# First batch of the FFT stages: A and the first tile's B moved from SBUF to SBUF instead of through memory

## What is computed

```python
# x: (4, 3008, 256); filt_r, filt_i: (1505, 256)
X = np.fft.rfft(x, axis=1)
y = np.fft.irfft(X * (filt_r + 1j * filt_i)[None], n=3008, axis=1)
x = y.reshape(12032, 256)
x = np.maximum(x @ w_in, 0.0) ** 2 @ w_out            # d_ff 2048
g = x @ w_gate                                        # d_ff 1536
out = (g / (1 + np.exp(-g)) * (x @ w_val)) @ w_out2
```

## Time and profile before

| | |
|---|---|
| median of 3 runs | 2358.94 us (2358.81 to 2359.14) |
| the profiled execution | 2358.64 us; span of its trace 2356.8 us |
| mean granted TensorE clock | 0.997 of full speed |
| TensorE (PE) busy | 2329.5 us, 99% of the span |
| weight loads (PEld) | 1903.6 us, 81% |
| VectorE, ScalarE, GpSimd busy | 68%, 54%, 3% |
| DMA | 153.74 MB, mean 65 GB/s |

### The profile page before, as it was taken

The page is one execution under the profiler, slowest core; times in us unless marked ns, Lnnn a source line. Parts: engine busy times, 40 slices in busy tenths (PEclk is TensorE's granted clock), DMA queues, the critical chain, the costliest instruction groups (busy, mean ns, idle before and its releaser), DMA issues.

```text
span 2356.8 us, 31292 instructions
## 1 busy us (share of the span) xinstructions
PE 2329.5 (99%) x10581; PEld 1903.6 (81%) x10581; DVE 1601.1 (68%) x2707; ACT 1272.7 (54%) x2468; POOL 61.2 (3%) x124
## 2 busy tenths in 40 slices
PE   8899999999999999999999999999999999999999
PEld 4688888888888888888888878888888888888887
DVE  3567766677666776566555777777777777777776
ACT  4566656566655665555544445555555555555554
POOL 0100000000000000000000000000000000000000
PEclk9899999999999999999999999999999999999999
DMA  9643433333333333101002101001011011010000
GB/s 270 207 132 96 129 96 107 91 107 112 101 98 99 99 106 122 29 27 42 27 19 72 50 1 36 23 14 36 1 36 36 1 36 36 1 36 28 10 19 18
DMA packets 95423, 153.74 MB, mean 65 GB/s; under 512 B 10080, under 2 KB 48416, under 8 KB 94976
## 3 DMA queue, kind: packets, MB, share of 16 engines
q1 hardware_dynamic: 82112, 132.96, 17.9%
q0 software_dynamic: 13152, 18.78, 3.3%
HBM read 101.89 MB, written 49.81 MB: 64 GB/s over the span
## 4 chain that ended last, share of the span: by engine, by line
PE 96%; DMA 2%; SPq 1%; ACT 1%; issue 1%; DVE 1%; POOL 0%; ACTq 0%; DVEq 0%
PE psum L1450 31%; PE psum L1452 31%; PE psum L1451 31%; PE psum L1552 1%; DMA filt0b<-filt 1%; PE psum L1554 1%; PE psum L1461 1%; DMA B_scratch<-b_out 0%; SPq L562 0%; SPq L557 0%; PE psum L1504 0%; DMA w<-w_full 0%; ACT turned L820 0%; DMA A_scratch<-a_out 0%; ACT z_raw L820 0%
## 5 line engine op out<-in xcount | busy, mean ns | idle before, releaser
L1217 DVE SCALAR_TENSOR_TENSOR prod<-psum,act_out 128x512 f32<-128x512 f32 (+1 forms) x384 | 260.9, 679 | 398.4 <-ACT act_out L917 397.9
L917 ACT ACTIVATE act_out<-psum 128x512 f32<-128x512 f32 (+1 forms) x384 | 226.1, 589 | 461.5 <-PE psum L1452 461.2
L1450 PE MATMUL psum<-g_hi,m_hi 128*128 128x512 f32 (+1 forms) x768 | 305.7, 398 | 2.0 <-ACT z_raw L820 1.8
L1450 PE MATMUL psum<-v_hi,m_hi 128*128 128x512 f32 (+1 forms) x768 | 297.7, 388 | 1.5 <-DVE v_lo L1115 1.5
L1452 PE MATMUL psum<-v_hi,m_lo 128*128 128x512 f32 (+1 forms) x768 | 296.7, 386 | 0.0
L1451 PE MATMUL psum<-v_lo,m_hi 128*128 128x512 f32 (+1 forms) x768 | 296.7, 386 | 0.0
L1452 PE MATMUL psum<-g_hi,m_lo 128*128 128x512 f32 (+1 forms) x768 | 296.5, 386 | 0.0
L1451 PE MATMUL psum<-g_lo,m_hi 128*128 128x512 f32 (+1 forms) x768 | 296.4, 386 | 0.0
L1115 DVE TENSOR_TENSOR g_lo<-prod,g_hi 128x512 fp32r<-128x512 f32 (+1 forms) x408 | 270.6, 663 | 1.1 <-ACT g_hi L820 1.0
L820 ACT ACTIVATE g_hi<-prod 128x512 fp32r<-128x512 f32 (+1 forms) x408 | 248.5, 609 | 0.9 <-DVE prod L1251 0.9
L1450 PE MATMUL psum<-g_hi,m_out 128*128 128x512 f32 (+1 forms) x576 | 226.0, 392 | 0.3 <-DVE g_lo L1115 0.3
(11 more groups left out here) (125 smaller groups left out, 4246.9 us busy)
## 6 DMA issues: line engine op xcount, KB each, us to landing
filt_in<-filt SPq DMA_DIRECT2D x36, 512.0 KB, 3.9
z_scratch<-z_raw SPq DMA_DIRECT2D x23, 512.0 KB, 2.9
b_in<-B_scratch SPq DMA_DIRECT2D x122, 96.0 KB, 2.8
zq_raw<-z_scratch SPq DMA_DIRECT2D x44, 256.0 KB, 3.5
B_scratch<-b_out SPq DMA_DIRECT2D x38, 256.0 KB, 2.1
A_scratch<-a_out SPq DMA_DIRECT2D x50, 192.0 KB, 2.1
x_in<-x SPq DMA_DIRECT2D x48, 192.0 KB, 2.8
a_in<-A_scratch SPq DMA_DIRECT2D x36, 256.0 KB, 3.3
```

Of the source, the lines that this page charges most:

```text
L917: nc.scalar.activation(act_out[n % 2][:, 0:w], psum[:, n % 3, 0:w], ACT.Relu).then_inc(relu_done, 1)
L1217: nc.vector.scalar_tensor_tensor(out=prod[n % 2][:, 0:w], in0=psum[:, n % 3, 0:w], scalar=0.0, in1=act_out[n % 2][:, 0:w], op0=ALU.max, op ...
L1450: nc.tensor.matmul(dst, wh, vh, start=start, stop=False, skip_group_check=True)
```

## The change

A of batch 0 no longer goes through `A_scratch`. As soon as ScalarE has copied a pair of positions, SP issues one DMA for each of the two positions p, from the 96 rows of `a0_out[:, p, :]` to the four partitions p, p + 32, p + 64 and p + 96 of `a0`, whose rows hold 24 x 256 numbers. For that the stage-1 table of batch 0 is reordered on the host, so that the 96 rows of A come in the order (r, k2) instead of (k2, r), and `a0_out` is one tensor of all 32 positions. The first `s2_0` waits for all 32 DMAs. The first filter load comes after the twelfth pair, the other five after all of A.

For B, the inverse table `inv` is reordered so that the rows of the first 6 positions of each group come first (24 rows), and the others after them (104 rows). For each unit SP issues two DMAs of the 24 rows from the copy's buffer to `b0_in` (4 partitions by 6 positions); POOL stores the other 104 rows of all 12 units in a scratch tensor of its own, which `load_b` reads later. `copy_b0` waits for both before it writes a buffer again. The eight weight loads follow the moves of the units 0 to 3, two each, and `keep_busy` has 5 and 4 products instead of 9 and 7.

```diff
-    w1_full = w1.reshape(PGS // 2, 2, PAIR, QP, ROWS).transpose(0, 3, 1, 2, 4)
+    w1_full = w1.reshape(PGS // 2, 2, PAIR, QP, K2, 4).transpose(0, 3, 1, 2, 5, 4).reshape(PGS // 2, QP, 2, PAIR, ROWS)
...
-    w23_full = np.concatenate([fwd, swapped, inv, turn], 1)
+    rows = np.arange(P).reshape(P // NP, NP)
+    first = np.concatenate([rows[:, 0:PAIR * G0].reshape(-1), rows[:, PAIR * G0:].reshape(-1)])
+    w23_full = np.concatenate([fwd, swapped, inv[:, first], turn], 1)
...
-    B_d = nc.dram_tensor("B_scratch", [B, UPS, P, PAIR, D], F32, kind="Internal").ap()
+    R = P // NP
+    HERE, REST = PAIR * G0, NP - PAIR * G0
+    B0_d = nc.dram_tensor("B0_scratch", [UPS, R * REST, PAIR, D], F32, kind="Internal").ap()
+    B_d = nc.dram_tensor("B_scratch", [B - 1, UPS, P, PAIR, D], F32, kind="Internal").ap()
...
-        x0, at = place(W_IN * PIECE * 4, "x0", [QP, NP, D])
-        assert at <= m1_lo_at + W_IN * PIECE * 4
-        a0_out = [place(m1_lo_at + W_IN * PIECE * 4, "a0_out0", [ROWS, NP // 2, D])[0],
-                  place(0, "a0_out1", [ROWS, NP // 2, D])[0]]
+        a0_out, at = place(0, "a0_out", [ROWS, NP, D])
+        assert at <= m1_lo_at
+        x0, at = place(m1_lo_at, "x0", [QP, NP, D])
+        assert at <= m1_end
...
-        def b_rows(b, k):
-
-            return B_d[b, :, :, k, :].rearrange("u (r p) d -> (u r) p d", p=NP)
+        def b_rows(b, k, lo, hi):
+
+            if b == 0:
+                return B0_d[:, :, k, :].rearrange("u (r p) d -> (u r) p d", p=REST)[:, lo - HERE:hi - HERE, :]
+            return B_d[b - 1, :, :, k, :].rearrange("u (r p) d -> (u r) p d", p=NP)[:, lo:hi, :]
...
-            def store_a0(n):
-                lo, hi = A_CUTS[n], A_CUTS[n + 1]
-                sp.wait_ge(a0_copied, hi)
...
-            def load_a0(n):
-                lo, hi = K_CUTS[n], K_CUTS[n + 1]
-                if n == 0:
-                    sp.wait_ge(a0_stored, 16 * (len(A_CUTS) - 1))
...
+            def move_a0(j):
+                sp.wait_ge(a0_copied, j + 1)
+                for p in range(PAIR * j, PAIR * (j + 1)):
+                    sp.dma_start(a0[p:P:NP, :, :], a0_out[:, p, :]).then_inc(a0_moved, 16)
...
-            def store_last_b0(u):
...
-            def load_b0(n):
...
-            def load_last_b0():
...
+            def move_b0(u):
+                sp.wait_ge(b0_copied, u + 1)
                 for k in range(PAIR):
+                    rows = slice(PAIR * R * u + k, PAIR * R * (u + 1), PAIR)
+                    sp.dma_start(b0_in[rows, :, :], b0_out[u % 4][0:R * HERE, k, :]).then_inc(b0_moved[u % 4], 16)
...
-            for n in range(len(A_CUTS) - 1):
-                store_a0(n)
-            load_filter0(0)
-            for n in range(3):
-                load_a0(n)
+            for j in range(PGS):
+                if j == 12:
+                    load_filter0(0)
+                move_a0(j)
             for n in range(1, len(FILT_CUTS) - 1):
                 load_filter0(n)
-                if n + 2 < len(K_CUTS) - 1:
-                    load_a0(n + 2)
             sp.dma_start(w4_0[:, :, :, :], w4_full).then_inc(w4_0_loaded, 16)
-            load_w_in(0)
-            load_w_out(0)
-            for n in range(UPS // 2 - 2):
-                load_b0(n)
-            store_last_b0(UPS - 2)
-            load_b0(UPS // 2 - 2)
-            store_last_b0(UPS - 1)
-            load_last_b0()
-            sp.wait_ge(b0_last_loaded, 16 * PAIR)
-            for k in range(1, 4):
-                load_w_in(k)
-                load_w_out(k)
+            for u in range(UPS):
+                move_b0(u)
+                if u < 4:
+                    load_w_in(u)
+                    load_w_out(u)
...
-                pool.dma_start(B_d[0, u], b0_out[u % 4][:, :, :]).then_inc(b0_stored[u % 4], 16)
+                pool.dma_start(B0_d[u], b0_out[u % 4][R * HERE:, :, :]).then_inc(b0_stored[u % 4], 16)
...
-            for u in range(UPS - 2):
+            for u in range(UPS):
                 store_b0(u)
...
                     act.wait_ge(b0_stored[u % 4], 16 * (u // 4))
+                    act.wait_ge(b0_moved[u % 4], 16 * PAIR * (u // 4))
...
-                if PAIR * u in K_CUTS:
-                    pe.wait_ge(a0_loaded[K_CUTS.index(PAIR * u)], 16)
+                    pe.wait_ge(a0_moved, 16 * NP)
...
-                    pe.wait_ge(b0_loaded, 16 * (UPS - 2))
-                    pe.wait_ge(b0_last_loaded, 16 * PAIR)
+                    for h in range(4):
+                        pe.wait_ge(b0_moved[h], 16 * PAIR * UPS // 4)
...
-            keep_busy(9)
+            keep_busy(5)
...
-            keep_busy(7)
+            keep_busy(4)
```

More of the change, by code:

```diff
@@ L300, in build @@
         a0_copied = sem("a0_copied")
-        a0_stored = sem("a0_stored")
-        a0_loaded = [sem(f"a0_loaded{n}") for n in range(len(K_CUTS) - 1)]
+        a0_moved = sem("a0_moved")
         s2_0_done = sem("s2_0_done")
@@ L308, in build @@
         b0_stored = [sem(f"b0_stored{k}") for k in range(4)]
-        b0_loaded = sem("b0_loaded")
-        b0_last_stored = [sem(f"b0_last_stored{k}") for k in range(2)]
-        b0_last_loaded = sem("b0_last_loaded")
+        b0_moved = [sem(f"b0_moved{k}") for k in range(4)]
         s4_0_done = sem("s4_0_done")
@@ L623, in load_b @@
                     for h in range(4):
-                        sp.wait_ge(b0_stored[h], 16 * -(-(UPS - 2 - h) // 4))
-                    for h in range(2):
-                        sp.wait_ge(b0_last_stored[h], 16)
+                        sp.wait_ge(b0_stored[h], 16 * UPS // 4)
                 elif i == 0:
```

23 lines of the change are left out of this document (3 added, 20 removed).

## The result

| | before | changed |
|---|---|---|
| median | 2359.04 us (2358.81 to 2360.88, 4 runs) | 2414.26 us (2407.80 to 2419.75, 4 runs) |
| the profiled execution, its span | 2358.64, 2356.8 us | 2413.01, 2411.2 us |
| mean granted clock | 0.997 | 0.984 |

The ratio is 1.0231 (95% interval 1.0205 to 1.0258): **slower by 55 us**, 18 more than forecast and 2 beyond the upper end of the range. The changed kernel's own four runs spread over 12 us, against 2 (other sets of runs of the kernel before, of 13 to 26 runs, spread over 5 to 8).

What follows compares the result with a forecast made beforehand. TensorE was taken as busy 99% of the span, losing time only in the first batch. `s4_0` at 120.0 instead of 77.45 gave +42.5, less 5.0 coming back, +37.5 on 2358.6: 2396 us, range 2360 to 2412.

Steps and rivals of the forecast that it cites:

- What bounds the kernel: TensorE is busy 99% of the span; long waits lie only before 77.45 us, in the first batch.
- Four engines: Each A move, 96 source rows to 4 partitions, runs on four DMA engines, each carrying 786 KB.
- the first rival: Source side decides, so A's moves use sixteen engines: A in at 27 to 34 us, total 2344; chance 0.17.
- 13.6 GB/s an engine: Rate of each engine in A's moves, from earlier loads with 1 KB rows; the moves take 57.8 us.
- the second rival: Four engines at full 26.8 GB/s each: A in place at 50.9 us, total 2366; chance 0.20.
- A in place at 80.6: A ready for `s2_0` at 19.8 + 57.8 + 2.4 + 0.6 = 80.6 us, against 32.2 before.
- the other filters stand behind A ... so they cost nothing: Remaining filter loads, on A's engines, need 2.4 us each, one consumed every two units (5.1 us): no cost.
- The stage: s2/s3 at 2.57 us a unit: 33.7 us, plus 2.3 for 4.6 us at half clock.
- covered, barely; if not, up to 3 us: ScalarE's copy of B waits for a move behind eight weight loads: 10 to 19 us against 20.6 available.
- B's last move, 3.4 us: Two small moves of 24 rows before `s4_0`, priced like the earlier last loads; lower bound 1.3 us.
- What comes back, -5.0: Short pause keeps full clock: `s4_0` takes 2.7 us instead of 5.4, first `up1` products 2.3 instead of 4.6.
- The slow end: A's moves at 10.7 GB/s an engine and a late clock: 2415 us; chance 0.04.

Runs made afterwards that it cites:

- e1: Changed kernel with the four destination rows of each A move on b, b+4, b+8, b+12 instead of p, p+32, p+64, p+96; 2385.98 us.
- e3: Changed kernel with A's moves issued by POOL and rows laid out so that successive moves land in different partition groups; 2379.93 us.
- e10: e8 with POOL's loads of its tables behind B's last move; 2402.97 us, ratio 1.0179 to the kernel before.
- e8: Changed kernel with SP waiting for all moves of A before issuing the other five filter loads; 2407.86 us.
- e16: e10 with eight filler products instead of four ahead of `s4_0` and two behind it; 2401.86 us.
- e13: Kernel before the change with 17 filler products instead of 7 ahead of `s4_0`; 2362.16 us, ratio 1.0017.
- e14: Kernel before the change with 17 filler products instead of 7 ahead of `s4_0` and two behind it; 2363.73 us, ratio 1.0022.
- e15: Only B moved, by POOL and for the last four units by SP, weights spread, POOL's tables held back, fillers on both sides of `s4_0`; 2359.82 us.
- e17: e14 with six weight loads issued behind B's later part, without the wait for B's last load; 2356.45 us, ratio 0.9984 to the kernel before.
- e18: e15 with its last four weight loads behind x and B's later part; 2356.33 us, ratio 0.9982 to the kernel before.
- e9: A through memory as before the change, only B moved, by POOL, six weights behind B's last move; 2362.17 us.
- e11: e9 with the six weights loaded from the copy of unit 9 on; 2360.99 us, ratio 1.0003 to the kernel before.

## Why the prediction was right, and where it failed

- **What bounds the kernel**: right. The whole loss lies before x's first product (53.4 of 54.4 us).
- **Four engines**: right (share 27.5%, 4 small packets a move). Sixteen engines as the first rival is out.
- **13.6 GB/s an engine**: the number was right (14), and that it was is in part luck: the sum took it from the earlier trace rows as the rate of an engine with rows of 1 KB, and e1 moved the same rows with the same engines at 24. What limits is where the rows land, as e1 and e3 show, a reason that stands in the prediction only beside the sum; one change of layout brought the second rival near (24 GB/s an engine, though A at 60.3 and not at 50.9).
- **A in place at 80.6**: right for the moves (78.5 to 81.9 in the three kernels that hold the filters back), failed in the changed kernel (85.4) at the step "the other filters stand behind A ... so they cost nothing". Issued behind is not carried out behind: they use the other engines as well, and disturb the last moves. +4.8 us.
- **The stage**: 2.57 us a unit, right. The clock was back after 6.1 us, not 4.6, so 3.0 instead of 2.3; ScalarE's second wait, "covered, barely; if not, up to 3 us", was not covered: 2.4. With 1.7 us that the stage itself took less, for which no cause was looked for, +1.4 (37.4 instead of 36.0).
- **B's last move, 3.4 us**: failed; 8.0 from the end of the last copy (122.79) to `s4_0` (130.78), +4.6. The loads of the earlier trace rows had the engines to themselves; this one shared them with POOL's stores and tables (without the tables, in e10, it took 1.3 us less than in e8). An estimate from an idle stretch was used for a busy one.
- **What comes back, -5.0**: the failed step with the largest price. Nothing came back: from `s4_0` to x's product it was 15.5 us, as before (15.4): +5.1. The pause without work was 6.05 us instead of 1.3, long enough for the clock to fall, at 129.0. The step was wrong also by itself: with a pause of 2.8 us (e10) the clock fell during `s4_0`, and only 2.4 of the 5.0 us came back. Fillers on both sides (e16) bring back 4.8 in the profile.
- Behind x's product 1.0 us more. Together 4.8 + 1.4 + 4.6 + 5.1 + 1.0 = 16.9, which is 2413.0 - 2396.1.

The chance of 0.80 on slower was on the right side, and of the likeliest case's mechanism the four engines, the long wait for A and the pace of the stage held; the reason of the rate and the -5.0 did not. The range was too narrow at the top: each of four terms was taken at its undisturbed value, and all four erred the same way. "The slow end" (2415) was nearly the measured time, for reasons other than its own.

## What to carry to other kernels

A move inside SBUF is not cheap because it spares a trip through memory; with 4 partitions on one side it was slower. Count the partitions and the groups that the destination rows fall in before counting bytes, and price every transfer with the neighbours it will really have. When a wait is taken away and nothing is gained, look for the next load behind the same queue's bulk: here one small load behind 2 to 3 MB of weights swallowed what the fillers saved in e13, e14 and e15. And look at the clock behind the new wait: in these three it fell there, so the saving turned into a loss or into nothing. In these kernels it held from `s4_0` to x's product only with fillers on both sides of `s4_0` and no long wait behind up1 (e16, e17, e18).

## What the runs showed of the hardware

- Four rows of 1 KB to p, p+32, p+64, p+96 moved at 56 GB/s, to b, b+4, b+8, b+12 at 96, from the same four engines at the same share (27.5 and 27.2%). A busy share says nothing about bytes: POOL's moves (69.9% share) moved 0.81 MB in 16 us, SP's (27.5%) 0.89.
- The granted clock fell 4.3 to 5.2 us after the last filler whether TensorE then stood (changed kernel, 124.7 to 129.0) or ran `s4_0` after a short pause or none (e10, 123.3 to 128.5; e13, 77.8 to 82.4). With two fillers right behind `s4_0` (e14, e16) it stayed up there. In e14 it then fell 2.9 us after TensorE's last product (87.3 to 90.2). What decides it was not measured.
- The time in which a 24 KB move of B (24 rows of 1 KB) lands depends on what runs beside it: 2.5 us in e9, 4.2 in e10, 5.8 in the changed kernel, 7.4 in e11.
